# Sending the whole third set of weights of the second mixture before the list of tiles is read

## The reference, cut to what matters

```python
def _moe2_ref(x, w_skip, w_gate, w1, w2):        # x (1536, 512), 8 experts, w1 (8, 512, 1024), w2 (8, 1024, 512)
    do_compute = x @ w_skip > 0
    out = x.copy()
    xc = x[do_compute]
    logits = xc @ w_gate
    e_idx = np.argmax(logits, axis=1)            # one expert for each row
    gate_w = softmax(logits)[row, e_idx]
    for e in range(8):
        mask = e_idx == e
        h = np.maximum(xc[mask] @ w1[e], 0.0)
        y[mask] = gate_w[mask, None] * (h @ w2[e])
    out[do_compute] = xc + y
```

## Time and profile before

| | us |
|---|---|
| median of 3 runs | 727.56 (725.95 to 727.91) |
| the profiled execution's own time | 727.6 |
| its span, first to last instruction | 725.9 |
| TensorE busy in the span | 703.0 |
| last pass's rows out | about 600.8 |
| all list entries in DRAM | 616.0 |
| layer 1 of the fourth tile begins | 626.1 |
| layer 1 of the seventh tile begins | 652.0 |
| from one layer 1 to the next, from the seventh tile to the last | 8.14 each |

### The profile page before, as it was taken

The page is one execution under the profiler, slowest core; times in us unless marked ns, Lnnn a source line. Parts: engine busy times, 40 slices in busy tenths (PEclk is TensorE's granted clock), DMA queues, the critical chain, the costliest instruction groups (busy, mean ns, idle before and its releaser), DMA issues.

```text
span 725.9 us, 12345 instructions
## 1 busy us (share of the span) xinstructions
PE 703.0 (97%) x4499; PEld 580.9 (80%) x4500; DVE 403.5 (56%) x1041; ACT 281.5 (39%) x654; POOL 66.2 (9%) x97
## 2 busy tenths in 40 slices
PE   6599999999999999999999999999999999999997
PEld 5488898898989889988988998899899885444443
DVE  4887584552795684754757364456437317443431
ACT  4745364451345434631621451054036112542430
POOL 2512000000000000000000000100010103233221
PEclk9989999999999999999999999999999999999999
DMA  9985632120708817723977738134630996699900
GB/s 210 213 201 114 135 81 57 39 48 4 287 3 327 333 62 268 295 75 93 427 286 295 261 116 346 63 114 158 247 117 1 361 375 233 242 395 396 375 3 22
DMA packets 92384, 139.36 MB, mean 192 GB/s; under 512 B 55172, under 2 KB 55456, under 8 KB 90656
## 3 DMA queue, kind: packets, MB, share of 16 engines
q1 hardware_dynamic: 89664, 133.89, 53.2%
q0 software_dynamic: 2656, 4.66, 2.0%
HBM read 104.05 MB, written 34.98 MB: 192 GB/s over the span
## 4 chain that ended last, share of the span: by engine, by line
PE 86%; DMA 5%; DVE 3%; issue 2%; SPq 1%; POOL 1%; ACT 1%; POOLq 0%; DVEq 0%
PE ps L1738 15%; PE ps L1740 15%; PE ps L1739 15%; PE ps L1988 8%; PE ps L1990 8%; PE ps L1989 8%; PE ps L2127 4%; PE ps L2099 4%; DMA sets<-in_moe_w 3%; PE ps L1800 2%; PE ps L1772 1%; PE ps L1786 1%; PE ps L1931 1%; DMA v_first<-stage 1%; PE ps L1751 1%
## 5 line engine op out<-in xcount | busy, mean ns | idle before, releaser
L1988 PE MATMUL ps<-xt_hi,wb_hi 128*128 128x384 f32 x336 | 112.7, 336 | 0.0
L1990 PE MATMUL ps<-xt_hi,wb_lo 128*128 128x384 f32 x336 | 112.4, 334 | 0.0
L1989 PE MATMUL ps<-xt_lo,wb_hi 128*128 128x384 f32 x336 | 112.3, 334 | 0.0
L969 ACT ACTIVATE h_raw<-ps 128x384 f32<-128x384 f32 x96 | 47.1, 490 | 116.2 <-PE ps L1990 114.0
L1739 PE MATMUL ps<-v_lo_acc,hb_hi 128*128 128x512 f32 x216 | 84.2, 390 | 0.0
L1365 DVE SCALAR_TENSOR_TENSOR acc<-ps,dp,acc 128x512 f32<-128x512 f32 x36 | 27.0, 750 | 99.3 <-PE ps L1740 99.3
L1350 DVE TENSOR_TENSOR h_raw<-ps,h_raw 128x384 f32<-128x384 f32 x96 | 49.7, 553 | 44.4 <-PE ps L1990 44.3
L975 ACT ACTIVATE hb_hi<-h_raw 128x384 fp32r<-128x384 f32 x96 | 49.0, 525 | 52.5 <-DVE h_raw L1350 52.5
L1988 PEld LDWEIGHTS ps<-xt_hi,wb_hi 128*128 128x128 f32 x336 | 63.1, 188 | 0.4
L1989 PEld LDWEIGHTS ps<-xt_lo,wb_hi 128*128 128x128 f32 x336 | 63.1, 188 | 0.3
L1990 PEld LDWEIGHTS ps<-xt_hi,wb_lo 128*128 128x128 f32 x336 | 63.1, 188 | 0.0
(11 more groups left out here) (269 smaller groups left out, 1301.0 us busy)
## 6 DMA issues: line engine op xcount, KB each, us to landing
sets<-in_moe_w SPq DMA_DIRECT2D x72, 512.0 KB
w_aside<-wb_hi SPq DMA_DIRECT2D x3, 3584.0 KB, 17.0
w_aside<-wb_lo SPq DMA_DIRECT2D x3, 3584.0 KB, 24.8
wb_hi<-w_aside SPq DMA_DIRECT2D x21, 512.0 KB, 10.8
wb_lo<-w_aside SPq DMA_DIRECT2D x21, 512.0 KB, 11.6
acc<-in_moe_w SPq DMA_DIRECT2D x12, 768.0 KB, 5.3
w_raw<-in_moe_w SPq DMA_DIRECT2D x12, 512.0 KB, 5.4
stage<-in_k SPq DMA_DIRECT2D x16, 192.0 KB, 4.1
```

Source lines behind the costliest of these rows:

```text
L969: nc.scalar.activation(h_raw[:, f, half * GT:(half + 1) * GT], ps[:, bank, 0:GT], ACT.Copy).then_inc(put_by, 1)
L1988: mm(to, wb_hi[w], hi(c), start=(c == 0 and not onto), stop=False, skip_group_check=onto)
L1989: mm(to, wb_hi[w], lo(c), start=False, stop=False, skip_group_check=onto)
L1990: last = mm(to, wb_lo[w], hi(c), start=False, stop=(c == HALF_D - 1), skip_group_check=onto)
```

## The change

The fourth piece of set 3's w1 and all of its w2 (five pieces of 512 KB, 2.62 MB) are issued directly behind the first three pieces, ahead of the waits for sets 1 and 2 and for the list's entries. Nothing is sent any more between the reading of the list and the loop. The wait for the gather of the fourth tile's rows stays; what follows it now is set 4.

```diff
             load_set(0, 1, range(1, 2))
             load_set(1, 1, range(3, PIECES))
-            load_set(3, 0, range(3))
+            load_set(3, 0)
+            load_set(3, 1)
             for e in (1, 2):
                 for layer in range(2):
                     arrived(e, layer)
...
             for j in range(SIDES):
                 sp.dma_start(lst[...], route_list...).then_inc(list_in, 16)
 
-            load_set(3, 0, range(3, PIECES))
             sp.wait_ge(list_in, 16 * SIDES)
             sp.wait_ge(gathered[STARS + 1], 16)
-            load_set(3, 1)
             for e in range(3, E2 + 1):
```

## The result

The changed kernel took 728.26 us in the median of 20 runs (726.82 to 731.34), the kernel before 726.35 us (724.46 to 728.22, 20 runs). The ratio is 1.0028, 95% interval 1.0018 to 1.0038: slower by 2.0 us (1.3 to 2.8). Two later timings of the same two kernels gave 1.0053 (1.0036 to 1.0069) and 1.0038 (1.0024 to 1.0052), that is +3.9 and +2.8 us. In all three the change is a loss, clear of the noise and under 1%; why the three differ by up to 1.9 us no run settles. The forecast was 728.1, with a range of 725.9 to 730.4.

What follows compares the result with a forecast made beforehand. TensorE was taken to bound the stage. Profiled execution 727.6, plus 1.9 us of waiting at the fourth tile, minus 1.4 at the seventh, gave 728.1; range 725.9 to 730.4.

Steps and rivals of the forecast that it cites:

- The bound of the gain: TensorE's wait for set 5 at the seventh tile: its removal gives back 1.4 to 1.55 us and no more.
- The weights: Five pieces issued early: stream ends at 620.7, set 4 follows the gather with both layers, seventh tile's wait goes, gain 1.4.
- (a): Last scatter's list entries, slowed by the weight stream: in DRAM at 619.6 instead of 616.0.
- the rule's sum: Sum if queues are served in turn packet by packet, entries in at about 616: said to be 0.4 us lower.
- (b): SP's list reads stand behind the weights on its queue: list in at 623.2, late by 2.8 us (1.9 to 4.5).
- (c): Fourth tile's gathered rows land at 626.95; after 0.9 us of slack PE waits 1.9 us.
- the sum: Profiled execution 727.6, plus 1.9 at the fourth tile, minus 1.4 at the seventh: 728.1.
- The list is not delayed: Rival: list reads come past the weights or the stream ends by 618, no new wait, 726.1; chance 0.14.
- Delayed more: Rival: list late by over 4.5 us, as when scatters wait for the stream's end, 731 to 732; chance 0.14.

Runs made afterwards that it cites:

- e7: Kernel before with three of the five pieces sent ahead of the waits and the list, the other two behind the gather; ratio 1.0012.
- e5: Changed kernel with its five pieces sent between the wait for the entries and the two list reads; ratio 1.0099 to the kernel before.
- e6: Kernel before with all five pieces behind the list reads and ahead of the wait for the gather; ratio 1.0042.
- e2: Changed kernel with the two list reads issued by ScalarE on its own DMA queue instead of SP; ratio 1.0024 to the kernel before.
- e1: Changed kernel with 16 turns of the identity on TensorE in its wait ahead of the fourth tile; ratio 1.0024 to the kernel before.
- p2: Changed kernel with the 16 identity turns again, timed beside the changed kernel on one chip; median 728.47, ratio 1.0022 to the kernel before.
- n1: The kernel before, unchanged, run again as a timing control and for a second trace; ratio 1.0001.
- e3: Kernel before with only the fourth piece of set 3's w1 ahead of the waits, all of w2 behind the gather; ratio 1.0007.

## Why the prediction was right, and what it had wrong

- **The bound of the gain** (1.38 us at the seventh tile, no more) held in the trace: the bracket is absent in each trace of the changed kernel. What I took from one trace as a property of the kernel is a wait that one of the two traces of before has, the one with the later list read. As a mean this term is too large.
- **The weights.** Ten pieces in a row on SP, done by 609.95 (I wrote about 612); stream to a little past 621 (620.7); set 4 with both layers back to back at 627.18 (about 627). Nothing was held on SP.
- **(a) The entries.** I took 5.7 us from issue to landing, it was 5.32; in DRAM at 618.97 (619.6). The sign and the size were right, from the lag of the first three scatters. The Trainium skill's rule (DMA: Bandwidth & Descriptors, Queues, rings and completion order) of queues served in turn packet by packet would have had them in at about 616; three traces of the changed kernel and e7 say 5.3 to 5.8 us under the stream, e5 and e6 2.1 without it. That the packets of both queues move side by side does fit the trace (q0's 32 with q1 at 102.5%); the lag lies ahead of them. (By my own numbers the rule's sum is 0.5 us lower and not 0.4: 623.2 less 622.7.)
- **(b) The list.** In at 623.36, I wrote 623.2. That the reads end with the stream came out (in some 2 us behind its end in the changed kernel and e2, 1.7 in e5). The reason that I gave, their place in SP's queue, is not shown: on ScalarE's queue they were no earlier (e2). Whether "(a) hardly matters" is true stays open, since no run has the entries in time with the same stream ahead of the reads. e7 shows that the stream at the reads alone is worth about 1.3 us.
- **(c) The fourth tile.** Wait of 1.9 us forecast; 2.28, 2.10 and 2.78 measured. The order of events was right.
- **The term that was missing.** Nothing in the sum stood for PE's clock. Behind the new idle time PE ran at the lower level for about 3 us, and from the turn of the rows to the end of layer 1 it took 1.4 to 1.6 us more (6.10, 6.23 and 6.02 us for 4.63). With a gain that is between 0 and 1.4 us by execution, and a wait 0.2 to 0.9 longer than forecast, it makes the difference between +0.5 and the +2.0 to +3.9 that were measured. e1 and p2 show it by taking it away. The lower clock was not looked for among the consequences of a wait, although a wait was forecast.
- **Rivals.** "The list is not delayed" fell at once. "Delayed more" did not occur either: from the third tile's turn to DVE's first id it is 4.5 us in the earlier trace rows's trace (616.05 to 620.56) and 7.7, 7.5 and 8.2 in the three of the changed kernel, a delay of 2.9 to 3.7, inside the 1.9 to 4.5 of the forecast. Against n1, the other trace of before, in which it is 3.35, the delay is 4.1 to 4.9, at and just over the forecast's end. The extra time over the sum came from the clock and from the wait that n1 does not have.

Two errors (a gain counted whole, a clock not counted) made the forecast too low by 1.5 us or more: it says +0.5 for a measured +2.0. A third pushed the other way. The forecast was added to 727.6, near the median of three executions, and the median of twenty is 726.35, 1.2 us lower. So the 0.2 us between 728.1 and 728.26 is luck. The sum's own range was -0.4 to +2.2: the +2.0 lies just inside it, the +3.9 and +2.8 of the later timings outside. The chain from entries to list to gather to PE's wait was right; the size of the loss was not.

## What to carry to other kernels

A hole in the DMA stream is not free room when a chain of small dependent transfers runs through it: each link that met the full stream took some 3 to 4 us more here: scatter (5.3 to 5.8 for 2.1), list read (6.3 for 2.6) or gather (6.6 for 2.6), on the queue of the weights or on GpSimd's. Count what the engine that then waits loses afterwards too: for TensorE an idle time of 2.1 to 2.8 us cost another 1.4 to 1.7 at the lower clock. And a wait of 1 us seen in one trace is worth a second trace before a gain is counted on it.

## What the runs showed of the hardware

- A scatter of 128 entries of 8 bytes took 2.1 us to land on idle queues and 5.3 to 5.8 us beside a stream of weights on another queue; a gather of a tile's rows 2.6 and 6.6 us.
- The lag of a scatter beside the stream lies ahead of its packets: in the changed kernel they moved 4.3 to 4.9 us behind the issue, with the stream at its full share; in e3 1.5 to 2.1 us behind it, as the stream ended (share of q1 0.40 in 616.25 to 616.5). What holds them is not settled; it is not simply the last packet of the stream.
- TensorE's idle times of 2.10, 2.28, 2.28, 2.40, 2.78 and 6.04 us were each followed by the lower clock; those of 0.61, 0.67, 0.83, 1.38 and 1.44 by none. Behind 2.78 and 6.04 the turn of the rows ran slow as well (0.68 and 0.69 us for 0.44).
